# Routing with a running sum of the experts' rounded counts, and other edits around the two routing stages

## The chip, the cores and the metric

The kernel runs on one core of a Trainium2 chip. The metric is the device time of one execution in microseconds (us). A core has TensorE (PE, matmuls; its weight loads are shown as PEld), VectorE (DVE), ScalarE (ACT), GpSimd (POOL) and SyncE (SP), each with its own instruction stream, which meet only at semaphores. The suffix q (DVEq, SPq) marks the sequencer of an engine: register work, branches, waits and DMA issues.

## The reference

Attention for 2 batches x 8 heads with 1152 keys; queries are pooled by two first, so that 576 rows per batch leave it. The result x, 1152 tokens x 512, passes two mixtures of experts:

```python
q_pool = q.reshape(B, H, S // 2, 2, D).mean(axis=3)
attn = softmax(scale * q_pool @ k.T); x = (attn @ v) as [tokens, heads * D]

# first mixture: top-1 of 8 experts, at most cap = 288 tokens for each
logits = x @ w_gate; e = argmax(logits); gate = softmax(logits)[e]
out[i] = gate[i] * (relu(x[i] @ w1[e]) @ w2[e])      # a token past the capacity gives 0

# second mixture: only tokens with x @ w_skip > 0, no capacity
out[i] = x[i] + gate[i] * (relu(x[i] @ w1[e]) @ w2[e])   # other tokens: out[i] = x[i]
```

## The kernel before

Everything is float32, or float32 split in two rounded parts. There are three kinds of stage.

**Attention.** Nine query tiles of 128 rows, head by head. The last head of the loop (`head(H - 1, 1, last=True)`, L852 for PE, L1316 for DVE) ends with the product of probabilities and V in PSUM, which DVE copies to `OT` in one instruction (`copy_output`, L1200); PE turns it back to token rows and takes the gate logits of this head along (`turn_back`, L780); DVE scales both (`output_logits` L1225, `output_x` L1232). `add_logits` (L1244, two reductions) sums the logits over heads, and stands after the last `copy_output`. SP writes each head's columns of x to DRAM with four DMAs (`store_x`, L441: the full tiles and the half tile of either batch), and waits for both of DVE's `output_x` of the head before the first of them.

**Routing, for m = 0 and m = 1** (L857 on PE, L1362 on DVE). Tokens are sorted by expert into tiles of 128 slots. Each expert's share is rounded up to grains of 64 slots, and a tile may hold two experts, so each tile is multiplied by a left and a right expert. DVE makes a one-hot of the expert of each token (`r_hot`). PE counts with it, by triangular and full matrices of ones, the place of every token in its expert and the total of each expert (`pos_ready`). DVE compares the totals with multiples of 64 (`r_cmp`, L1413), sums (`r_nt`), sums again over the experts before (`r_sq`, `r_base`), adds the place, and cuts the slot number in a tile number (`r_which`, `r_tile`) and a row (`r_inside`, `r_place`). POOL multiplies `r_tile` with the token numbers (`r_ids`, L655), PE finds with `r_place` the token of each slot (`rows_found`, L890), DVE writes the row numbers (`rows_in`, L1443), and POOL gathers the first 128 rows of x by an indirect DMA (L606). Beside it DVE and PE find the gates (`r_gcut`, `gates_cut`, L898), and DVE makes the tables of experts per tile (`tab_n`, `tab_done`, `tab_grain`, up to L1464), after which it copies the first right-hand weights (`fill_right`, L323). While PE waits it multiplies `ident` with itself (`keep_busy(n)`, L838, two records for each of the n in the profile).

**Experts** (L986 PE, L1143 ACT, L1481 DVE). For each tile: hidden product, relu, transposes, second product. x comes by POOL's gather, the weights by SP's DMAs of 512 KB in rings of four (first layer) and three (second layer). The row of SP's requests is written by hand: after attention it waits for the last x stores (L463), requests the second-layer weights of expert 0 (L464), waits for the first gathered x tile (L465), and requests more. DVE copies y out for all tiles but the last of m = 0, and takes the logits of the second router from it with nine products (L1355). The last tile of m = 0 goes another way: ACT copies y (L1163), PE turns it (`turn_y`, L975), ACT copies it again (L1165), PE multiplies with the router's weights (`next_logits`, L982), ACT copies the logits (L1167). In the meantime DVE leaves its loop over tiles (L1496, up to 12 passes, of which those past the last tile are skipped by a branch), loads `tab_n` in a register and waits for these logits (L1386). DVE then finds the active tokens, and the routing of m = 1 runs.

Of the kernel before, what the change touches and what calls it, by code (L numbers as in the profile page):

```python
# [37 lines left out]
def build(nc, q, k, v, gate1, w1_1, w2_1, skip_w, gate2, w1_2, w2_2, next_w, out, x_dram, cap):  # L38
# [15 lines left out]
    NCMP = B * SQ // GRAIN  # L54
# [11 lines left out]
    with ExitStack() as ctx:  # L66
# [20 lines left out]
        grain_steps = sb("grain_steps", [P, NCMP])  # L87
        iota_grain = sb("iota_grain", [P, NTAB])
        iota_slot = sb("iota_slot", [P, NSLOT])
        upto = sb("upto", [P, E, E])  # L90
        earlier = sb("earlier", [P, E, E])
# [58 lines left out]
        r_cmp = sb_in(moe, "r_cmp", [P, E, NCMP])  # L150
        r_nt = sb_in(moe, "r_nt", [P, E])
        r_sq = sb_in(moe, "r_sq", [P, E, E])
        r_endc = sb_in(moe, "r_endc", [P, E])
        r_over = sb_in(moe, "r_over", [P, NT, E])
        r_gcut = sb_in(moe, "r_gcut", [P, 2, NSLOT], F32R)
        r_base = sb_in(moe, "r_base", [P, E])
        r_slot = sb_in(moe, "r_slot", [P, NSLOT])
# [3 lines left out]
        r_drop = sb_in(moe, "r_drop", [P, NSLOT])  # L161
# [43 lines left out]
        tile_ready = sem("tile_ready")  # L205
# [21 lines left out]
        CONST_STEPS = 27  # L227
# [131 lines left out]
        def _(sp):  # L359
# [98 lines left out]
            store_x(H - 1)  # L458
# [45 lines left out]
        def _(pool):  # L504
# [60 lines left out]
            for dst, pattern, base in ((expert_rank, [[-1, E]], E), (grain_steps, [[GRAIN, NCMP]], 0),  # L565
                                       (iota_grain, [[1, NTAB]], 0), (iota_slot, [[1, NSLOT]], 0),
                                       (iota_p, [[1, P]], 0)):
                link(nc.gpsimd.iota(dst[:], pattern, base=base, channel_multiplier=0,
                                    allow_small_or_imprecise_dtypes=True))
            link(nc.gpsimd.memset(grain_steps[:, 0:1], -1.0))  # L570
            link(nc.gpsimd.memset(upto[:], 1.0))
            link(nc.gpsimd.affine_select(out=upto[:], in_=upto[:], pattern=[[1, E], [-1, E]], compare_op=ALU.is_ge,
                                         fill=0.0, base=0, channel_multiplier=0))
            link(nc.gpsimd.memset(earlier[:], float(GRAIN)))
            link(nc.gpsimd.affine_select(out=earlier[:], in_=earlier[:], pattern=[[1, E], [-1, E]],
                                         compare_op=ALU.is_gt, fill=0.0, base=0, channel_multiplier=0))
# [11 lines left out]
            for m in range(2):  # L588
# [34 lines left out]
                def store_y(t, count, last=False):  # L623
# [5 lines left out]
                    pool.wait_ge(y_copied, t + 1)  # L629
# [55 lines left out]
        def _(pe):  # L685
# [82 lines left out]
            def turn_back(b, h):  # L768
# [7 lines left out]
                pe.wait_ge(ot_copied, h * 2 + (b + 1))  # L776
# [76 lines left out]
            turn_back(1, H - 1)  # L853

            for m in range(2):
# [15 lines left out]
                pe.matmul(place_of(0, n), before[:], hot, start=True, stop=False, skip_group_check=True)  # L871
                if m == 0:
# [11 lines left out]
                keep_busy((18, 19)[m], HID_BANK + 1)  # L884
# [16 lines left out]
                keep_busy((16, 12)[m], HID_BANK + 1)  # L901
# [70 lines left out]
                def turn_y(t):  # L972
                    pe.wait_ge(y_copied, t + 1)
                    for c in range(DC):
                        mm = pe.transpose(bank(YT_BANK)[:, c * P:(c + 1) * P], ylast[:, c * P:(c + 1) * P], ident[:])  # L975
                    mm.then_inc(y_turned, 1)

                def next_logits():

                    pe.wait_ge(yt_ready, 1)  # L980
                    for c in range(DC):
# [26 lines left out]
                if m == 0:  # L1008
                    keep_busy(2, HID_BANK + 1)
                    turn_y(rest + 1)  # L1010
                    keep_busy(2, HID_BANK + 1)
                    next_logits()
# [3 lines left out]
        def _(act):  # L1016
# [92 lines left out]
            for m in range(2):  # L1109
# [62 lines left out]
        def _(dve):  # L1172
# [21 lines left out]
            def copy_output(b, h):  # L1194
# [5 lines left out]
                nc.vector.tensor_copy(OT[:, b, :], bank(PV_BANK)).then_inc(ot_copied, 1)  # L1200
# [55 lines left out]
            def head(h, par, last=False):  # L1256
# [35 lines left out]
                copy_output(1, h)  # L1292
# [24 lines left out]
            add_logits(0, H)  # L1317
            add_logits(1, H - 1)
# [43 lines left out]
            for m in range(2):  # L1362
# [31 lines left out]
                hot = nc.vector.tensor_tensor(of(r_hot), of(r_rank), per_expert(r_best), ALU.is_equal)  # L1394
                if m == 1:
                    link(hot)
                    hot = nc.vector.tensor_tensor(of(r_hot), of(r_hot), per_expert(active), ALU.mult)
                hot.then_inc(hot_ready, 1)

                if m == 1:  # L1400
                    link(nc.vector.tensor_scalar(r_drop[:], active[:], -float(OUT_OF_RANGE), float(OUT_OF_RANGE),
                                                 ALU.mult, ALU.add))
# [8 lines left out]
                grains = min(-(-cap // GRAIN), NCMP) if m == 0 else NCMP  # L1411
                cmp = r_cmp[:, :, 0:grains]
# [5 lines left out]
                pos = psum[:, 0, 0:n * E].rearrange("p (t e) -> p t e", e=E)  # L1418
                if m == 0:
                    link(nc.vector.tensor_scalar(r_over[:], pos, float(cap), float(OUT_OF_RANGE), ALU.is_ge, ALU.mult))  # L1420
                tt(of(r_pos), pos, per_tile(r_base, E), ALU.add)
                if m == 0:
                    tt(of(r_pos), of(r_pos), r_over[:], ALU.add)
                tt(of(r_pos), of(r_pos), of(r_hot), ALU.mult)
                if m == 0:
                    with nc.allow_low_precision(reason="whole numbers far below 2 ** 24"):
                        reduce(of(r_whole), of(r_pos), ALU.add)
                else:
                    reduce(of(r_slot), of(r_pos), ALU.add)
                    tt(of(r_whole), of(r_slot), r_drop[:], ALU.add)  # L1430
# [112 lines left out]
```

## Time and profile before

| what | us |
|---|---|
| median of 3 runs | 618.69 |
| lowest, highest | 618.34, 618.9 |
| the profiled execution | 618.62 |
| its span, first to last instruction | 616.9 |
| PE busy | 594.9 (96%) |
| DVE busy | 315.1 (51%) |
| ACT busy | 266.9 (43%) |
| mean share of full TensorE clock granted | 0.995 |

Times in the views count from the first instruction. Attention ends on PE near 273 us, the first routing lasts to about 291 us, the experts of m = 0 to 446.6 us, the second routing to 466.5 us, and the experts of m = 1 to the end. A row that says busy tells how long the engine had an instruction in work, not that the end of the kernel depends on it.

### The profile page before, as it was taken

What the parts mean: (1) busy time and instruction counts of PE and PEld (TensorE: products, weight loads), DVE (VectorE), ACT (ScalarE), POOL (GpSimd) and SP (SyncE); (2) the same over time, 40 slices, a digit from 0 to 9 for tenths busy, and PEclk for the clock granted to TensorE, in tenths of its full rate; (3) what the DMA queues carried; (4) which work ended last, traced back from release to release, by engine and by line L of the source; (5) the groups of instructions that cost most, each with busy time, mean ns of one, the idle gap of its engine ahead of it and who ended that gap; (6) DMA issues with size and microseconds to landing.
All of it is one profiled execution on the core that took longest, in us unless ns stands there. A gap on an engine that the chain in (4) does not pass through costs nothing.

```text
span 616.9 us, 12447 instructions
## 1 busy us (share of the span) xinstructions
PE 594.9 (96%) x3719; PEld 352.3 (57%) x3720; DVE 315.1 (51%) x666; ACT 266.9 (43%) x439; POOL 191.5 (31%) x168
## 2 busy tenths in 40 slices
PE   8899999999999999998999999999999999999993
PEld 7677787877777777777333333333395333333331
DVE  5457565657575756656355652965574220322220
ACT  4655565655565656520244444444102444444410
POOL 4785635344453800001012221122211122222222
PEclk9999999999999999999999999999999999999997
DMA  8979818171721062006999397780846798841111
GB/s 201 291 184 258 186 39 173 39 166 45 153 50 26 11 232 87 22 9 208 399 391 409 124 352 275 284 307 29 305 174 229 274 312 322 321 150 43 45 52 61
DMA packets 42637, 111.61 MB, mean 181 GB/s; under 512 B 16020, under 2 KB 16020, under 8 KB 41536
## 3 DMA queue, kind: packets, MB, share of 16 engines
q1 hardware_dynamic: 38528, 99.03, 50.5%
q0 software_dynamic: 4080, 12.22, 5.7%
q8 instruction: 15, 0.25, 0.2%
q14 instruction: 14, 0.11, 0.1%
HBM read 102.68 MB, written 12.06 MB: 186 GB/s over the span
## 4 chain that ended last, share of the span: by engine, by line
PE 90%; DMA 2%; DVE 2%; issue 2%; ACT 2%; POOLq 0%; POOL 0%; SPq 0%; DVEq 0%; ACTq 0%
PE psum L929 41%; PE psum L704 14%; PE psum L718 11%; PE psum L752 9%; PE psum L916 4%; PE psum L838 3%; PE psum L780 3%; PE psum L764 1%; PE psum L748 1%; DMA xraw<-moe_in,rows_in 1%; DVE probs L1181 1%; ACT probs L1019 1%; PE psum L931 1%; DMA qraw<-in_q_dram 1%; DMA res<-moe_in,idx_r 1%
## 5 line engine op out<-in xcount | busy, mean ns | idle before, releaser
L929 PE MATMUL psum<-w1ring,XT 128*64 x304 | 134.5, 595 | 0.8 <-ACT XT L1126 0.4
L929 PE MATMUL psum<-w2ring,HT 128*64 x304 | 133.7, 592 | 1.7 <-DVE wright L323 1.7
L931 PE MATMUL psum<-wright,XT 128*64 128x512 f32 x304 | 134.5, 595 | 0.0
L931 PE MATMUL psum<-wright,HT 128*64 128x512 f32 x304 | 133.7, 592 | 0.0
L1181 DVE TENSOR_SCALAR_CACHE_REDUCE probs<-psum 128x1152 f32<-128x1152 f32 x72 | 97.5, 1357 | 62.6 <-PE psum L704 62.6
L1019 ACT ACTIVATE probs<-probs,nmax 128x1152 f32<-128x1152 f32 x72 | 90.7, 1260 | 45.6 <-DVE probs L1181 45.6
L704 PE MATMUL psum<-KT,QT 128*128 128x384 f32 x480 | 102.0, 350 | 3.0 <-DVE probs L1181 1.7
L929 PEld LDWEIGHTS psum<-w2ring,HT 128*64 128x64 f32 x304 | 41.5, 137 | 87.3 <-issue 87.3
L704 PEld LDWEIGHTS psum<-KT,QT 128*128 128x128 f32 x480 | 80.2, 188 | 15.0 <-issue 7.9
L929 PEld LDWEIGHTS psum<-w1ring,XT 128*64 128x64 f32 x304 | 40.1, 137 | 79.8 <-issue 79.8
L718 PE MATMUL psum<-ident,probs 128*128 128x128 f32 x648 | 82.0, 275 | 1.1 <-ACT probs L1019 0.6
L718 PEld LDWEIGHTS psum<-ident,probs 128*128 128x128 f32 x648 | 72.7, 140 | 9.2 <-issue 3.7
L1133 ACT ACTIVATE hid<-psum,slot_gate 128x1024 f32<-128x1024 f32 x19 | 21.2, 1114 | 125.2 <-PE psum L931 125.2
L1026 ACT COPY PT<-psum 128x512 f32<-128x512 f32 x88 | 48.4, 588 | 60.3 <-PE psum L718 60.3
L752 PE MATMUL psum<-PT,V 128*64 128x512 f32 x256 | 62.2, 605 | 0.0
L323 ACT COPY wright<-w1ring 128x1024 f32 x60 | 58.1, 1040 | 0.0
L323 DVE COPY wright<-w2ring 128x1024 f32 x76 | 49.1, 700 | 14.3 <-DMA w2ring<-in_moe_w_dram 14.2
L1348 DVE TENSOR_TENSOR orow<-psum,res 128x512 f32<-128x512 f32 x9 | 6.2, 691 | 97.0 <-PE psum L931 88.1
L1355 DVE CUSTOM_DVE_ANT_0 psum<-ysb,wnext 128x512 f32<-128x512 f32 x81 | 52.9, 723 | 0.0
L595 POOL COPY idx_x<-rows_in 128x1 int32 x15 | 8.8, 585 | 142.0 <-PE psum L916 142.0
L335 POOL CAST KT<-kraw 128x2304 fp32r<-128x2304 f32 x7 | 14.7, 2106 | 87.3 <-PE psum L704 82.8
L931 PEld LDWEIGHTS psum<-wright,HT 128*64 128x64 f32 x304 | 41.5, 137 | 0.0
(169 smaller groups left out, 645.7 us busy)
## 6 DMA issues: line engine op xcount, KB each, us to landing
w1ring<-in_moe_w_dram SPq DMA_DIRECT2D x64, 512.0 KB, 6.9
w2ring<-in_moe_w_dram SPq DMA_DIRECT2D x64, 512.0 KB, 7.1
qraw<-in_q_dram SPq DMA_DIRECT2D x30, 288.0 KB, 10.0
kraw<-in_k_dram SPq DMA_DIRECT2D x14, 576.0 KB, 9.2
V<-in_v_dram SPq DMA_DIRECT2D x8, 576.0 KB, 4.0
moe_in<-zero SPq DMA_DIRECT2D x9, 256.0 KB, 3.1
wnext<-in_next_w_dram SPq DMA_DIRECT2D x1, 2304.0 KB, 17.1
out_dram<-moe_in SPq DMA_DIRECT2D x1, 2304.0 KB, 9.4
```

Source lines behind the costliest of these rows:

```text
L323: copy(wright[k][:, part * PIECE:(part + 1) * PIECE], piece_of(k, slot, part).rearrange("p o f -> p (o f)")).then_inc(filled, 1)
L704: mm = pe.matmul(dst, QT[par][:, piece, q0:q0 + P], KT[par][:, b * S + c * KB:b * S + (c + 1) * KB], start=(i == 0), stop=(i == 2 * len(pa ...
L718: mm = pe.transpose(bank(T_BANK + place % 3)[:, i * P:(i + 1) * P], src, ident[:])
L752: mm = pe.matmul(psum[rows, PV_BANK, :], V[par][:, b * KT_N + j, :], PT[:, j, :], start=(j < 2), stop=False, skip_group_check=True)
L916: return pe.matmul(place[:, chunk * P:(chunk + 1) * P], src, ident[:], is_transpose=True, start=first, stop=False, skip_group_check=True)
L929: pe.matmul(psum[0:GRAIN, b, :], lhs[:, c * P:c * P + GRAIN], left, start=first, stop=last, skip_group_check=True)
L931: return pe.matmul(psum[GRAIN:P, b, :], lhs[:, c * P + GRAIN:(c + 1) * P], wright[k][:, cols], start=first, stop=last, skip_group_check=True)
L1019: nc.scalar.activation(probs[:, t, :], probs[:, t, :], ACT.Exp, bias=nmax[:, t:t + 1], scale=-1.0, accum_out=den[:, t:t + 1]).then_inc(pro ...
L1026: nc.scalar.copy(dst, bank(T_BANK + place % 3, cols)).then_inc(turned_by_act, 1)
L1133: nc.scalar.activation(hid[:].rearrange("p (c f) -> p c f", c=2), psum[:, HID_BANK:HID_BANK + 2, :], ACT.Relu, scale=g).then_inc(relu_read ...
L1181: nc.vector.tensor_scalar(probs[:, t, :].rearrange("p (c k) -> p c k", c=3), scores_in(h, t), -SCALE, None, ALU.mult, ALU.min, accum_out=n ...
L1355: nc.vector.tensor_tensor_reduce(out=bank(JUNK_BANK + e % 2), in0=ysb[:], in1=wnext[:, e, :], scale=1.0, scalar=0.0, op0=ALU.mult, op1=ALU ...
```

## The change

The grain count is rounded by float arithmetic: `half_grain` adds 31.5 to each expert's total on PE, and a running sum (`tensor_tensor_scan`) that starts at ROUND + P, where neighbouring floats are 64 apart, gives the rounded ends of all experts in one instruction. `grain_steps`, `upto`, `earlier` and the arrays made from them are gone. Capacity is cut by a mask on the one-hot; slots are counted from P, so that a token that is left out gets 0 and meets no tile. Five counts of `keep_busy` shrink. The last head's `OT` is copied in two halves, three of the four last x stores are issued when their rows are written, the last y tile is copied in halves, and DVE instead of ACT copies the turned y and its logits. SP's requests after the x stores are as before: the second-layer weights of expert 0 come ahead of the wait for the first x.

```diff
-            store_x(H - 1)
+            last_rows = token_rows(x_dram[0])
+            for i, written in ((0, 2 * H - 1), (1, 2 * H - 1), (3, 2 * H - 1), (2, 2 * H)):
+                sp.wait_ge(x_written, written)
+                parts, tiles, rows = last_rows[i]
+                sp.dma_start(rows[:, :, (H - 1) * D:H * D], xpair[parts, tiles, :]).then_inc(x_stored, 16)
...
-                    pool.wait_ge(y_copied, t + 1)
+                    if last:
+                        pool.wait_ge(ylast_copied, 2)
+                    else:
+                        pool.wait_ge(y_copied, t + 1)
...
+                if last:
+                    pe.wait_ge(ot_part, 1)
+                else:
+                    pe.wait_ge(ot_copied, h * 2 + (b + 1))
...
+                    if last and n == 2:
+                        pe.wait_ge(ot_copied, h * 2 + (b + 1))
...
+                pe.matmul(place_of(n, n + 1), whole[:], half_grain[:].unsqueeze(1), start=False, stop=False, skip_group_check=True)
...
-                keep_busy((18, 19)[m], HID_BANK + 1)
+                keep_busy((14, 14)[m], HID_BANK + 1)
...
-                keep_busy((16, 12)[m], HID_BANK + 1)
+                keep_busy((8, 8)[m], HID_BANK + 1)
...
+                def turn_y():
+
+                    for i in range(2):
+                        pe.wait_ge(ylast_copied, i + 1)
+                        for c in range(2 * i, 2 * i + 2):
+                            mm = pe.transpose(bank(YT_BANK + i)[:, c * P:(c + 1) * P], ylast[:, c * P:(c + 1) * P], ident[:])
+                        mm.then_inc(y_turned, 1)
+
+                def next_logits():
+
                     for c in range(DC):
+                        if c % 2 == 0:
+                            pe.wait_ge(yt_ready, c // 2 + 1)
                         mm = pe.matmul(bank(LG_BANK, E + 1), yT[:, c * P:(c + 1) * P], wcat[:, c, :],
...
-                    nc.scalar.copy(ylast[:], bank(Y_BANK)).then_inc(y_copied_[0], 1)
-                    act.wait_ge(y_turned, 1)
-                    nc.scalar.copy(yT[:], bank(YT_BANK)).then_inc(yt_ready, 1)
-                    act.wait_ge(lg_done, 1)
-                    nc.scalar.copy(logits2[:, bass.ds(rest + 1, 1), :].rearrange("p o c -> p (o c)"), bank(LG_BANK, E + 1)
-                                   ).then_inc(lg_copied, 1)
+                    for i in range(2):
+                        half = slice(i * 2 * P, (i + 1) * 2 * P)
+                        nc.scalar.copy(ylast[:, half], bank(Y_BANK)[:, half]).then_inc(ylast_copied, 1)
...
+                if last:
+                    add_logits(0, H)
+                    add_logits(1, H - 1)
+                copy_output(1, h, last)
...
-                    link(nc.vector.tensor_scalar(active[:], logits2[:, :, E], 0.0, None, ALU.is_gt))
+                    nc.vector.tensor_scalar(active[:], logits2[:, :, E], 0.0, 2.0 * E, ALU.is_gt, ALU.mult).then_inc(active_ready, 1)
...
-                if m == 1:
-                    link(hot)
-                    hot = nc.vector.tensor_tensor(of(r_hot), of(r_hot), per_expert(active), ALU.mult)
+                if m == 0:
+                    hot = nc.vector.tensor_tensor(of(r_hot), of(r_rank), per_expert(r_best), ALU.is_equal)
+                else:
+                    dve.wait_ge(active_ready, 1)
+                    tt(of(r_best), of(r_best), active[:], ALU.add)
+                    hot = nc.vector.scalar_tensor_tensor(of(r_hot), of(r_rank), 2.0 * E, per_expert(r_best), ALU.add, ALU.is_equal)
...
-                tt(cmp, bc(tot.unsqueeze(2), [P, E, grains]), bc(grain_steps[:, 0:grains].unsqueeze(1), [P, E, grains]), ALU.is_gt)
-                reduce(r_nt[:], cmp, ALU.add)
-                tt(r_sq[:], bc(r_nt[:].unsqueeze(1), [P, E, E]), earlier[:], ALU.mult)
-                reduce(r_base[:], r_sq[:], ALU.add)
+                half = (GRAIN - 1) / 2.0
+                link(nc.vector.tensor_scalar(r_held[:], tot, float(cap if m == 0 else B * SQ) + half, 1.0 + half, ALU.min, ALU.max))
+                link(nc.vector.tensor_tensor_scan(ends[:, 1:E + 1], r_held[:], r_held[:], ROUND + P, ALU.add, ALU.max))
...
-                    link(nc.vector.tensor_scalar(r_over[:], pos, float(cap), float(OUT_OF_RANGE), ALU.is_ge, ALU.mult))
-                tt(of(r_pos), pos, per_tile(r_base, E), ALU.add)
+                    nc.vector.scalar_tensor_tensor(of(kept), pos, float(cap), of(r_hot), ALU.is_lt, ALU.mult).then_inc(kept_ready, 1)
+                link(nc.vector.scalar_tensor_tensor(of(r_pos), per_tile(ends[:, 0:E], E), ROUND, pos, ALU.subtract, ALU.add))
...
-                    reduce(of(r_slot), of(r_pos), ALU.add)
-                    tt(of(r_whole), of(r_slot), r_drop[:], ALU.add)
-                link(nc.vector.tensor_scalar(of(r_inside), of(r_whole), P - 1, None, ALU.bitwise_and))
+                nc.vector.tensor_scalar(of(r_inside), of(r_whole), P - 1, None, ALU.bitwise_and).then_inc(inside_ready, 1)
...
+                if m == 0:
+                    sum_gates()
                 dve.wait_ge(rows_found, m + 1)
                 found = psum[:, 7, 0:NSLOT]
                 nc.vector.tensor_scalar(rows_in[m][:, 0:NSLOT], found, -1.0, 0.0, ALU.add, ALU.max).then_inc(rows_in_ready, 1)
-                if m == 0:
-                    sum_gates()
...
-                tt(r_sq[:], bc(r_nt[:].unsqueeze(1), [P, E, E]), upto[:], ALU.mult)
-                reduce(r_endc[:], r_sq[:], ALU.add)
...
-                if m == 1:
+                if m == 0:
+                    for i in range(2):
+                        half = slice(i * 2 * P, (i + 1) * 2 * P)
+                        dve.wait_ge(y_turned, i + 1)
+                        nc.vector.tensor_copy(yT[:, half], bank(YT_BANK + i)[:, half]).then_inc(yt_ready, 1)
+                    at = bass.ds(rest + 1, 1)
+                    dve.wait_ge(lg_done, 1)
+                    nc.vector.tensor_copy(logits2[:, at, :].rearrange("p o c -> p (o c)"), bank(LG_BANK, E + 1)
+                                          ).then_inc(lg_copied, 1)
+                else:
                     copy_y(m, rest + 1)
```

## Rows read from the trace of the kernel before

**Rows 1.** The page's chain that ended last: share of the span by engine.

```profile
PE 90%; DMA 2%; DVE 2%; issue 2%; ACT 2%; POOLq 0%; POOL 0%; SPq 0%; DVEq 0%; ACTq 0%
```

**Rows 2.** Chain of waits through the first routing: start us, us, what.

```profile
271.61 0.70 DVE OT L1200
...
273.53 2.50 PE psum L838 x22
...
276.41 4.12 PE psum L838 x36
...
283.05 6.28 DMA xraw<-moe_in,rows_in
```

**Rows 3.** Timeline of DVE, first routing: start us, us, engine, line, what, xcount.

```profile
269.49 0.48 DVE L1232 TENSOR_TENSOR xpair<-psum,rden 128x320 f32<-128x320 f32 x1
...
274.42 0.23 DVE L1390 TENSOR_TENSOR r_diff<-logits,r_max 128x72 f32<-128x72 f32 x1
274.57 0.23 DVE L1335 TENSOR_TENSOR r_eq<-logits,r_max 128x72 f32<-128x72 f32 x1
...
276.45 0.20 DVE L1335 TENSOR_TENSOR r_cmp<-psum,grain_steps 128x40 f32<-128x40 f32 x1 [0.51 <-PE psum L867]
...
279.38 1.70 DVE L1437 TENSOR_TENSOR r_place<-iota_p,r_inside 128x384 fp32r<-128x384 f32 x3
...
281.94 0.22 DVE L1338 TENSOR_REDUCE r_sum<-r_exp 128x9 f32<-128x72 f32 x1
...
282.65 0.17 DVE L1446 CAST r_gcut<-gate 128x9 fp32r<-128x9 f32 x1
...
287.20 2.50 DVE L323 COPY wright<-w1ring 128x1024 f32 x4 [1.37 <-issue]
```

**Rows 4.** Timeline of SP, first routing: the last x stores, the weight request.

```profile
275.96 3.27 SPq L441 DMA_DIRECT2D moe_in<-xpair  x4
280.61 0.36 SPq L397 DMA_DIRECT2D w2ring<-in_moe_w_dram  x1
```

**Rows 5.** DMA issues, 275.9 to 276.1, then 277.9 to 278.6: us to landing last.

```profile
moe_in<-xpair SPq DMA_DIRECT2D x1, 128.0 KB, 2.0
...
moe_in<-xpair SPq DMA_DIRECT2D x1, 128.0 KB, 3.3
```

**Rows 6.** Chain of waits through the second routing.

```profile
448.59 1.06 PE psum L982 x8
...
452.89 4.35 PE psum L838 x38
...
462.46 2.77 PE psum L838 x24
```

**Rows 7.** Timeline of DVE, second routing.

```profile
449.98 0.17 DVE L1387 TENSOR_SCALAR active<-logits 128x14 f32<-128x14 f32 x1 [3.21 <-ACT logits L1167]
...
453.09 0.31 DVE L1335 TENSOR_TENSOR r_cmp<-psum,grain_steps 128x144 f32<-128x144 f32 x1
...
456.11 2.61 DVE L1437 TENSOR_TENSOR r_place<-iota_p,r_inside 128x384 fp32r<-128x384 f32 x5
```

**Rows 8.** DVE's sequencer, 446 to 450: count, ns, first and last start us.

```profile
L1496 DVEq ALU_OP  x5: 40/40/40, 446.6 to 448.9; - x5
L1386 DVEq TENSOR_LOAD <-tab_n x1: 317/317/317, 449.0 to 449.0; - x1
L1386 DVEq ALU_OP  x1: 40/40/40, 449.7 to 449.7; - x1
```

**Rows 9.** POOL's first gather of m = 1, and its us to landing.

```profile
460.59 1.08 POOL L606 DMA_INDIRECT xraw<-moe_in,rows_in  x1 [3.56 <-DVE rows_in L1443]
xraw<-moe_in,rows_in POOLq DMA_INDIRECT x1, 3.5
```

**Rows 10.** Windows after the last matmul: stretch, length, busy, PEclk, DMA share, GB/s.

```profile
607.00:608.00 1.00, 0.07 (x2) 0.00 (x0) 0.00 (x0) 0.00 (x0) 0.30 (x2) 1.00 0.35 49
...
610.50:611.00 0.50, 0.00 (x0) 0.00 (x0) 0.00 (x0) 0.00 (x0) 0.00 (x0) 0.68 0.00 0
```

More of the change, by code:

```diff
@@ L53, in build @@
     NSLOT = -(-NGRAIN // (2 * PER_TILE)) * 2
-    NCMP = B * SQ // GRAIN
+    ROUND = float(GRAIN * 3 << 22)
     KB = S // 3
@@ L86, in build @@
         expert_rank = sb("expert_rank", [P, E])
-        grain_steps = sb("grain_steps", [P, NCMP])
+        half_grain = sb("half_grain", [P, E], BF16)
+        ends = sb("ends", [P, E + 1])
         iota_grain = sb("iota_grain", [P, NTAB])
         iota_slot = sb("iota_slot", [P, NSLOT])
-        upto = sb("upto", [P, E, E])
-        earlier = sb("earlier", [P, E, E])
         wcat = sb("wcat", [P, DC, E + 1])
@@ L149, in build @@
         r_pos = sb_in(moe, "r_pos", [P, NSLOT, E])
[L150 to L154, printed above, removed]
+        r_held = sb_in(moe, "r_held", [P, E])
+        r_kept = sb_in(moe, "r_kept", [P, NT, E])
         r_gcut = sb_in(moe, "r_gcut", [P, 2, NSLOT], F32R)
-        r_base = sb_in(moe, "r_base", [P, E])
-        r_slot = sb_in(moe, "r_slot", [P, NSLOT])
         r_whole = sb_in(moe, "r_whole", [P, NSLOT], I32)
@@ L225, in build @@
         res_loaded = sem("res_loaded")
-        CONST_STEPS = 27
+        CONST_STEPS = 23
         START = 1
@@ L564, in _ @@
             link(nc.gpsimd.tensor_copy(into_upper[:], scratch[:]))
-            for dst, pattern, base in ((expert_rank, [[-1, E]], E), (grain_steps, [[GRAIN, NCMP]], 0),
-                                       (iota_grain, [[1, NTAB]], 0), (iota_slot, [[1, NSLOT]], 0),
+            for dst, pattern, base in ((expert_rank, [[-1, E]], E), (iota_grain, [[GRAIN, NTAB]], P),
+                                       (iota_slot, [[1, NSLOT]], 1),
                                        (iota_p, [[1, P]], 0)):
@@ L569, in _ @@
                                     allow_small_or_imprecise_dtypes=True))
[L570 to L576, printed above, removed]
+            link(nc.gpsimd.memset(half_grain[:], (GRAIN - 1) / (2.0 * P)))
+            link(nc.gpsimd.memset(ends[:, 0:1], ROUND + P))
             for b in range(B):
@@ L766, in attend_mid, with turn_back @@
                 mm.then_inc(mid_done, 1)
-            def turn_back(b, h):
+            def turn_back(b, h, last=False):
                 if b == 0:
@@ L852, in _ @@
             head(H - 1, 1, last=True)
-            turn_back(1, H - 1)
+            turn_back(1, H - 1, last=True)
             for m in range(2):
@@ L1192, in copy_tiles, with copy_output @@
                     copy_turned(h, turn_no(b, j))
-            def copy_output(b, h):
+            def copy_output(b, h, last=False):
                 u = h * 2 + b
@@ L1291, in head @@
                     maximum(h + 1, 3)
-                copy_output(1, h)
+                if last:
+                    add_logits(0, H)
+                    add_logits(1, H - 1)
+                copy_output(1, h, last)
             nc.vector.memset(qraw[0][:, :, SQ:SQ + P], 0.0).then_inc(pads_ready, 1)
@@ L1425, in _ @@
-                if m == 0:
-                    with nc.allow_low_precision(reason="whole numbers far below 2 ** 24"):
-                        reduce(of(r_whole), of(r_pos), ALU.add)
-                else:
-                    reduce(of(r_slot), of(r_pos), ALU.add)
-                    tt(of(r_whole), of(r_slot), r_drop[:], ALU.add)
-                link(nc.vector.tensor_scalar(of(r_inside), of(r_whole), P - 1, None, ALU.bitwise_and))
+                    dve.wait_ge(kept_ready, 1)
+                tt(of(r_pos), of(r_pos), of(kept), ALU.mult)
@@ L1432, in _ @@
+                with nc.allow_low_precision(reason="whole numbers far below 2 ** 24"):
+                    reduce(of(r_whole), of(r_pos), ALU.add)
+                nc.vector.tensor_scalar(of(r_inside), of(r_whole), P - 1, None, ALU.bitwise_and).then_inc(inside_ready, 1)
                 link(nc.vector.tensor_scalar(of(r_which), of(r_whole), 7, None, ALU.logical_shift_right))
@@ L1452, in _ @@
                 last.then_inc(gates_cut, 1)
-                tt(r_sq[:], bc(r_nt[:].unsqueeze(1), [P, E, E]), upto[:], ALU.mult)
-                reduce(r_endc[:], r_sq[:], ALU.add)
-                link(nc.vector.tensor_scalar(r_ends[:], r_endc[:], float(PER_TILE - 1), None, ALU.add))
-                link(nc.vector.tensor_scalar(r_tiles[:], r_ends[:], SHIFT, None, ALU.logical_shift_right))
+                link(nc.vector.tensor_scalar(r_ends[:], ends[:, 1:E + 1], ROUND + P, float(P - 1), ALU.subtract, ALU.add))
+                link(nc.vector.tensor_scalar(r_tiles[:], r_ends[:], 7, None, ALU.logical_shift_right))
                 link(nc.vector.tensor_scalar(tab_n[m][:], r_tiles[0:1, E - 1:E], -2.0, None, ALU.add))
-                tt(r_til[:], bc(iota_grain[:].unsqueeze(2), [P, NTAB, E - 1]),
-                   bc(r_endc[:, 0:E - 1].unsqueeze(1), [P, NTAB, E - 1]), ALU.is_ge)
+                link(nc.vector.scalar_tensor_tensor(r_til[:], bc(ends[:, 1:E].unsqueeze(1), [P, NTAB, E - 1]), ROUND,
+                                                    bc(iota_grain[:].unsqueeze(2), [P, NTAB, E - 1]),
+                                                    ALU.subtract, ALU.is_le))
                 reduce(r_tab[:], r_til[:], ALU.add)
```

34 lines of the change are left out of this document (11 added, 23 removed).

## The prediction

> **What bounds the kernel now.** I read the chain of waits first. PE holds 90% of it [rows 1], so an edit counts only where it lets PE go on earlier. The experts' stages are unbroken products and the diff leaves them alone; what it touches lies in the two routings. Next I read the chain through each of them. In the first it goes from DVE's last copy of the attention output at 271.61 over PE's filler (`keep_busy`, L838) to the first gather of x, 6.28 us from issue to landing, at 283.05 + 6.28 = 289.33 [rows 2]. In the second it is filler and small products throughout: 38 filler records to 452.89 + 4.35 = 457.24 and 24 more to 462.46 + 2.77 = 465.23 [rows 6]. There the gather landed at 460.59 + 3.5 = 464.1, before PE wanted it [rows 9]. So the first routing ends with a transfer, the second with a count of filler matmuls. One filler costs two records, 2 x 4.12 / 36 = 0.229 us [rows 2].
>
> Each routing is walked through below in times of the old trace.
>
> **First routing up to the gather.** (a) DVE copied `OT` from 271.61 in 0.70. Halves of 256 columns are not in the trace; 320 columns from PSUM took 0.48 [rows 3], and a line through 0.70 and 0.48 gives 0.41. PE can start after the first half, 0.70 - 0.41 = 0.29 earlier; I take 0.28. The bounds are 0, if a half cost as much as the whole, and 0.35. `add_logits`, moved ahead of the copy, falls in DVE's wait from 269.49 + 0.48 = 269.97 to 271.61. The turn and the 11 fillers that follow move with it, and so do the x rows of the last half head.
>
> (b) The one matmul of 8 columns for `half_grain` I take at 0.03, within 0 to 0.2. PE's totals come 0.25 earlier, so DVE's first operation on them stands at 276.20 in place of 276.45.
>
> (c) From there to the first `r_place` DVE took 279.38 - 276.45 = 2.93 [rows 3] for twelve small operations, nearly all waiting for the one before. An unlinked pair stands 0.15 apart (274.42, 274.57) and a linked one costs its duration and some 0.04. Now there are nine: the clamp 0.21, the scan, the mask 0.15 unlinked, place plus base 0.27, times mask 0.27, sum 0.26, `r_inside` 0.10 unlinked, `r_which` 0.21, `r_tile` 0.21. No row shows a scan. It has 8 elements; the nearest row, 40 elements of `r_cmp`, took 0.20, and 72 elements 0.23, so 0.25 with its link, bounds 0.2 and 0.6. Sum 1.93. `r_place` starts at 278.13.
>
> (d) PE had used `r_place` 1.15 after its start (276.41 + 4.12 = 280.53 against 279.38). With 14 fillers for 18 it comes free at 276.16 + 3.21 = 279.37, 1.24 after the new start, so the shorter filler uncovers nothing. `rows_found` is 1.16 earlier. `sum_gates`, 282.65 - 281.94 = 0.71 long [rows 3], goes into DVE's wait for it. POOL issues the gather at 283.05 - 1.17 = 281.88.
>
> **What the gather then waits for.** (e) The x stores: all four were issued from 275.96, over 3.27 us, and SP requested weights at 280.61, when the last had landed [rows 4]. The first full tile, issued with nothing ahead of it, landed in 2.0, a later one in 3.3 [rows 5]. Now three go out from 269.97 and have 5.7 us for it; only the last full one follows `output_x` at 275.96 - 0.28 = 275.68. With 2.0 it lands at 277.7, and the weight request moves to 277.75: 2.86 earlier (by 3.3: 1.6 earlier).
>
> (f) The weights' 2 MB and the gather's 0.26 MB fill the queues together until the gather lands, 289.33 - 280.61 = 8.72 after the first request. The gather alone needed 3.5 [rows 9]; the other 2.8 of its 6.28 is this traffic. If it still lands when all of it has drained, x is there at 277.75 + 8.72 = 286.5. If the queues shared fully, or the weights were gone, it lands at 281.88 + 3.5 = 285.4. The weights have been under way 4.1 us when the gather is issued, against 2.4 before, so a little less of them is in front: I take 286.3, 3.0 earlier.
>
> (g) PE's filler after the gates falls from 16 to 8 and ends near 284.7; PE then stands idle some 1.6 us until x comes. DVE's first weight copy started at 287.20 [rows 3]. It moves by 1.17 + 0.71 at least, to 285.3, and its first quarter (0.63) is ready at 285.9, before XT can be used near 287.9. The first hidden product is 3.0 earlier. The experts' weights are requested when x lands or when a ring slot is free; these requests move along.
>
> **Second routing.** (h) The turned y. Before, ACT copied it and PE's eight product records began at 448.59 and took 1.06 to 449.65 [rows 6]. Now DVE copies it, and DVE isn't there in time: its sequencer goes through the skipped passes of the loop over tiles until 448.9 + 0.1 = 449.0 [rows 8], a time set by the nine products with the last but one y and not by anything that the change shortens. It hid behind ACT's path; now it is the path. The copy of the first half goes 449.08 to 449.50, the second to 449.83; PE's products run from 449.54 in two halves of 0.53 to 450.60, 0.95 late. That ACT hands y over in halves gains nothing ahead of such a wait.
>
> (i) The register load. `tab_n` is loaded for the wait on the logits, from 449.0 to 449.74 [rows 8]; before, this too lay ahead of the logits, which came at 449.95. Now the load stands in program order behind DVE's own wait for PE and its copy. Copy at 450.70, load done at 451.44, `active` at 451.52 instead of 449.98 [rows 7]: 1.54 late. If the sequencer went on to the load without waiting, (i) would shrink to about 0.75.
>
> (j) From `active` to PE's totals took 452.89 - 449.98 = 2.91. `active` unlinked saves 0.1, one addition over 14 elements for a product over 112 saves 0.1, the extra matmul costs 0.03: 2.74, totals at 454.26, 1.37 late. `r_drop` is gone, so DVE, which came 0.20 after PE (453.09), is there with it, at 454.30. Its chain was 456.11 - 453.09 = 3.02 [rows 7] and is 0.21 + 0.25 + 0.31 + 0.31 + 0.30 + 0.10 + 0.21 + 0.28 = 1.97 by the same pricing: `r_place` at 456.27, 0.16 late. Fourteen fillers take PE from 454.26 to 457.47, 0.23 late; that covers `r_place` by 1.20 where it had 1.13.
>
> (k) The gather is issued at 460.59 + 0.23 = 460.82 and lands by 464.3. The gates' products end 0.23 late, at 462.69; 8 fillers for 12 take 1.85, to 464.54. That is 0.7 before 465.23. The gather is 0.2 ahead of it, so it isn't late. DVE's tables lose two operations and hold nothing up.
>
> **Sum.** 3.0 + 0.7 = 3.7 us. Against the profiled execution's 618.62 (span 616.9 and 1.7 around it; 0.07 below the median of the runs) this is 614.9 us. A difference of 0.2%, 1.2 us, is about what a measurement of this kernel can tell from none.
>
> **Rivals.** *The gather shares instead of draining.* x lands at 285.4, the first part gains 3.9, time 614.0. For it: most of the weights are gone by then. Against it: before, 0.26 MB took 2.8 us longer than alone and landed last. The Trainium skill ("DMA: Bandwidth & Descriptors", Queues, rings and completion order) has each engine alternate packet by packet between its queues, which is this rival's rule; the old trace doesn't bear it out as equal shares.
>
> *The stores land late.* If the last x store takes 3.3, the weights start 1.6 earlier only and x lands with them, at 287.7: 1.6 + 0.7 = 2.3, time 616.3. For it: the 3.3 of [rows 5]. Against it: that one was issued behind others.
>
> *DVE is in time.* If (h) and (i) cost nothing, the filler counts and the gather bound the second routing: everything to the gather's issue is 1.3 earlier, and x lands at 462.8, 2.3 before 465.2. Time 613.3. Against it: the loop's end at 449.0 is read, not assumed.
>
> *The clock falls (the slower side).* PE idles 1.6 us ahead of x, or up to 3.0 if the filler ends early and x comes at 287.7, where 16 fillers once bridged all but 0.9. After the last matmul the granted clock stayed at full speed from 607.1 to about 610.5 [rows 10], so 3.4 us of idling did not lower it there; this idle is shorter. If it does fall to 1.2 GHz, the first hidden product, 7.1 us, runs at half pace: 3.5 us if it recovers half way, 7 if not; with 5, 619.9. It decides from an added loss of 3.7. The Trainium skill ("TensorE: Matmul & The Clock Gate", HAM oscillation) names just such waits for a transfer between bursts as what brings the clock down; by it alone one would leave the fillers in. Rows 10 speak against it for this length.
>
> **How the numbers follow.** Forecast, 613.9 to 616.0 with its own errors: 0.55. Sharing gather 0.1, DVE in time 0.07, late stores 0.16, clock 0.07. The remaining 0.05 is for a loss I don't see, such as a scan at its upper bound together with a later ylast store, ending near no change. The forecast's unknowns, scan 0.2 to 0.6 twice, halves 0 to 0.35, reach to 616; with the late stores 617.0 is the upper end, with the other two 613.3 the lower. The first three and most of the late stores are faster by more than 1.2 us: 0.81. Within 0.2%: 0.11. Slower: 0.08.
>
> **What would show it.** In the profile after: SP's weight request near 277.8 (e); `r_place` 1.9 after the first operation on the totals (c); the first gather landing near 286.3, with PE idle ahead of it and a clock of 1.00 (f, g); DVE's copy of the turned y near 449.1 less 3.0, idle PE ahead of the products, and the load of `tab_n` behind the copy of the logits (h, i), each in the new trace's times; PE without a wait for x in the second routing (k). The distance from the last y product of m = 0 (446.6) to the second routing's end (465.2), 18.6 us, should be 17.9. The prediction is wrong if x lands with the weights unchanged, if the distance grows, or if a clock below 1.00 stands behind 284.

## The result

The changed kernel takes 619.70 us in the median of 13 runs (618.77 to 622.34), the kernel before 618.67 (617.99 to 619.81): ratio 1.0021, 95% interval 1.0011 to 1.0031. It is slower by 1.0 us where 3.8 less were forecast. The profiled execution took 618.77 us with a span of 617.0 and is the fastest of the 13. The mean granted clock is 0.988 to 0.993 in these runs, against 0.995 in the profiled execution before.

The chain of waits through the first routing, which answers to [rows 2]:

```profile
271.54 0.43 DVE OT L1204
...
273.19 2.50 PE psum L840 x22
...
276.10 3.23 PE psum L840 x28
...
281.85 6.46 DMA xraw<-moe_in,rows_in
...
290.02 1.05 PE psum L932
...
298.45 1.12 ACT hid L1139
```

The gather is issued 1.20 us earlier and still takes 6.46 us. The first matmul record of the hidden product is 1.05 long, where it was 0.64 before. PE's first instruction on x, and then the windows of this stretch (length, busy time of PE, PEld, DVE, ACT, POOL, then granted clock, DMA share, GB/s):

```profile
288.36 0.65 PE L919 MATMUL psum<-ident,xraw 128*128 128x128 f32 x4 [3.62 <-DMA xraw<-moe_in,rows_in]
...
284.00:285.00 1.00, 0.74 (x7) 0.55 (x5) 0.34 (x1) 0.00 (x0) 0.00 (x0) 1.00 1.01 401
...
287.00:288.00 1.00, 0.00 (x0) 0.00 (x0) 0.86 (x6) 0.00 (x0) 0.00 (x0) 1.00 0.47 189
288.00:289.00 1.00, 0.64 (x6) 0.65 (x7) 0.24 (x2) 0.00 (x0) 0.00 (x0) 1.00 0.00 0
289.00:290.00 1.00, 1.00 (x9) 0.78 (x7) 0.00 (x0) 0.65 (x2) 0.08 (x1) 0.59 0.63 119
...
291.00:292.00 1.00, 1.00 (x6) 0.34 (x4) 0.00 (x0) 0.00 (x0) 0.00 (x0) 0.50 0.88 307
292.00:293.00 1.00, 1.00 (x4) 0.16 (x2) 0.00 (x0) 0.00 (x0) 0.00 (x0) 0.70 1.00 410
```

PE ran out of fillers at 284.74 and stood idle for 3.62 us until x landed at 288.31. The clock then stood at 1.2 GHz from near 289.2 to 292.6, and the first hidden product lasted from 289.95 to 298.36, 8.4 us where it took 7.1 before. It begins 0.98 earlier and its end is 0.33 later than before, not 3.0 earlier.

DVE's chain, beside [rows 3], is as fast as hoped:

```profile
276.13 0.17 DVE L1418 TENSOR_SCALAR r_held<-psum 128x8 f32<-128x8 f32 x1 [0.54 <-PE psum L869]
276.33 0.18 DVE L1419 TENSOR_TENSOR_SCAN ends<-r_held 128x8 f32<-128x8 f32 x1
...
277.96 1.70 DVE L1439 TENSOR_TENSOR r_place<-iota_p,r_inside 128x384 fp32r<-128x384 f32 x3
```

SP and the last x store, beside [rows 4, 5]: the timeline, then the DMA issue of 275.6 to 276.4, then the packets of the hardware queue and of the instruction queue from 277.0 to 277.5, the instruction queue alone from 277.45 to 277.5, then the packets from 277.5 to 279.6.

```profile
269.92 6.08 SPq L457 DMA_DIRECT2D moe_in<-xpair  x4
279.79 10.38 SPq L392 DMA_DIRECT2D w2ring<-in_moe_w_dram  x8
...
moe_in<-xpair SPq DMA_DIRECT2D x1, 128.0 KB, 4.0
...
q1 hardware_dynamic: 132, 0.03, 27.1%
q8 instruction: 1, 0.02, 11.6%
...
q8 instruction: 1, 0.02, 116.0%
...
q1 hardware_dynamic: 33, 0.01, 3.1%
```

The last store landed 4.0 us after its issue, with no other store ahead of it. Of its 528 packets 495 had gone by 277.5; the other 33 came after 278. 528 packets over 16 DMA engines are 33 for each, so one engine's whole share was late. One packet of the instruction queue (a fetch of instructions, by the queue's name) began at 277.49. A share of 116.0% of 16 engines in 0.05 us is 0.93 us for it, so that it ended at 278.42; the first of the 33 late packets began at 278.40.

The second routing, DVE beside [rows 7, 9], then PE's wait for DVE's copy:

```profile
449.21 0.76 DVE L1504 COPY yT<-psum 128x256 f32<-128x256 f32 x2 [2.26 <-issue]
450.93 0.17 DVE L1507 COPY logits<-psum 128x9 f32 x1 [0.97 <-PE psum L988]
451.69 0.17 DVE L1395 TENSOR_SCALAR active<-logits 128x14 f32<-128x14 f32 x1 [0.59 <-DVE logits L1507]
...
456.56 2.62 DVE L1439 TENSOR_TENSOR r_place<-iota_p,r_inside 128x384 fp32r<-128x384 f32 x5
...
449.69 1.06 PE L988 MATMUL psum<-wcat,yT 128*128 128x9 f32 x8 [1.34 <-DVE yT L1504]
```

The last y product of m = 0 ends 0.14 later than before, so DVE's copy and `active` stand where they were forecast. PE waited 1.34 us for the copy; the clock stayed at 1.00 there. x landed 3.8 us after POOL's issue at 461.06, and PE turned it at 464.90: 0.17 earlier than before, from a start 0.14 later. The hidden product of m = 1 starts at 466.42, 0.13 earlier than before. By the end of the execution 0.3 us is lost again, and where was not followed up.

### The profile page after: what moved, and what is told of

The parts are those of the page before. It is cut to its first block, busy times and chain, and to the rows that moved or that the text cites. A ratio compares the mean times of both kernels' runs of the same rounds, so it can differ in the third digit from the quotient of the medians.

```text
span 617.0 us, 12355 instructions
## 1 busy us (share of the span) xinstructions
PE 591.3 (96%) x3679; PEld 348.0 (56%) x3680; DVE 312.1 (51%) x659; ACT 266.1 (43%) x438; POOL 190.6 (31%) x164
## 4 chain that ended last, share of the span: by engine, by line
PE 88%; DVE 4%; issue 3%; DMA 2%; ACT 2%; DVEq 0%; POOLq 0%; POOL 0%; SPq 0%; ACTq 0%
PE psum L932 40%; PE psum L701 14%; PE psum L715 11%; PE psum L749 9%; PE psum L919 4%; PE psum L782 3%; PE psum L840 2%; PE psum L761 1%; PE psum L745 1%; DMA xraw<-moe_in,rows_in 1%; DVE probs L1184 1%; ACT probs L1025 1%; PE psum L934 1%; DMA qraw<-in_q_dram 1%; DMA res<-moe_in,idx_r 1%
```

## The experiments

All times are medians; each ratio is against the kernel before, run on the same chip. Differences from the changed kernel are taken between medians of different chips; the kernel before had 618.56 to 618.70 on them.

**Fillers against the clock.** The changed kernel with 16:

```diff
-                keep_busy((8, 8)[m], HID_BANK + 1)
+                keep_busy((16, 8)[m], HID_BANK + 1)
```

> The changed kernel with 16 fillers instead of 8 behind the gates of m = 0 (8 stay for m = 1). Theory A, the clock: PE idled 3.6 us ahead of the first x, the clock fell to 1.2 GHz and the first hidden product took 8.4 us for 7.1. With 16 fillers the idle is 1.8 us, the clock stays at 1.00, x lands where it did, near 288.3: about 1.4 us less than the changed kernel, near 618.2 when before stands at 618.7. Rival B, the fillers don't matter and the whole change is a wash because the gather comes with the weights: same time as the changed kernel, 619.7, and the spread of its runs stays as wide.

618.33 us, ratio 0.9994 (0.9985 to 1.0003), 1.4 less than the changed kernel. The size is as expected, the reason isn't: PE idled only 1.93 us and the clock fell all the same, from 288.9. The two profiled executions, which both lost it, took the same time (618.75 and 618.77), so where the 1.4 of the medians comes from is not shown.

```profile
289.00:290.00 1.00, 1.00 (x6) 0.96 (x5) 0.00 (x0) 0.65 (x2) 0.12 (x1) 0.50 0.91 147
...
292.00:293.00 1.00, 1.00 (x8) 0.36 (x6) 0.00 (x0) 0.00 (x0) 0.00 (x0) 0.87 1.03 418
```

**The same cut in the kernel before**, 16 to 8 for m = 0 and nothing else:

```diff
-                keep_busy((16, 12)[m], HID_BANK + 1)
+                keep_busy((8, 12)[m], HID_BANK + 1)
```

> The kernel before with one number changed: 8 fillers instead of 16 behind the gates of m = 0. x still lands near 289.3, so PE idles some 2.7 us ahead of it. Theory A1, the clock falls after any idle of this kind: first hidden product 1.0 to 1.4 us longer, time 619.9. Theory A2, an idle of 2.7 us is still short enough and only the 3.6 of the changed kernel lost the clock: same time as before, 618.7, clock 1.00 through the stage. Which one holds tells whether the fillers alone, without the rest of the change, cost the time.

620.13 us, 1.0022 (1.0011 to 1.0033). PE idled 3.13 us ahead of x, and the clock was low from 290.4 to 293.9. Theory A1 holds: this number alone makes the kernel slower by as much as the whole change does. Of the 1.8 us by which the profiled execution is longer, 0.5 is no clock: x landed at 289.80 for 289.33. Of its 12 runs the two with a mean clock of 0.996 and 0.997 took 617.96 and 618.50; those at 0.989 took 621.2 to 621.8.

```profile
289.85 0.66 PE L916 MATMUL psum<-ident,xraw 128*128 128x128 f32 x4 [3.13 <-DMA xraw<-moe_in,rows_in]
```

**Enough fillers**, 24 in the changed kernel:

```diff
-                keep_busy((8, 8)[m], HID_BANK + 1)
+                keep_busy((24, 8)[m], HID_BANK + 1)
```

> The changed kernel with 24 fillers instead of 8 behind the gates of m = 0, enough to reach from 282.7 to the first x at 288.3 (8 left 3.6 us idle and 16 left 1.9, and both lost the clock). Theory A: the loss of the change lies in this idle alone; clock 1.00 to the tail, first hidden product 7.1 us for 8.4, and besides no run with a long low stretch: 617.6 to 618.1, with a spread under 1 us where the changed kernel has 3.6. Rival B: the clock is lost in the second routing's idle instead (PE waits 1.3 us for DVE's copy of the turned y), or something else takes the gain: 619 and more, wide spread.

618.01 us, 0.9994 (0.9986 to 1.0003), runs from 616.92 to 619.24. In the first routing theory A came true (clock 1.00 through, hidden product from 289.75). But rival B is right of the whole: now the clock fell in the second routing, behind PE's 1.34 us of waiting for DVE's copy of the turned y, and 11 fillers took 4.1 us for 2.7. From the turning of y (L980) to the hidden product of m = 1 it is 20.0 us, in the changed kernel's trace 19.2.

```profile
448.00:450.00 2.00, 1.74 (x11) 1.74 (x12) 0.71 (x3) 0.00 (x0) 0.00 (x0) 0.75 0.30 115
450.00:452.00 2.00, 2.00 (x11) 2.00 (x11) 1.36 (x6) 0.30 (x1) 0.00 (x0) 0.50 1.24 393
452.00:454.00 2.00, 2.00 (x29) 1.99 (x28) 1.05 (x5) 0.00 (x0) 0.00 (x0) 0.90 0.99 369
```

**ACT copies the turned y** and its logits in the changed kernel, halves kept:

```diff
-                        nc.vector.tensor_copy(yT[:, half], bank(YT_BANK + i)[:, half]).then_inc(yt_ready, 1)
...
+                        nc.scalar.copy(yT[:, half], bank(YT_BANK + i)[:, half]).then_inc(yt_ready, 1)
```

> The changed kernel with the two halves of the turned y and the logits of the last tile of m = 0 copied by ACT, as before, instead of by DVE. Theory A: DVE's late arrival and its register load cost some 1.5 us between the last y product of m = 0 and the second routing's active tokens; without them active stands near 450.1, place finding comes 1.5 us earlier, and the time falls by 1.3 to 1.5 us to near 618.3. The clock in m = 0 is still lost. Rival B, the fillers (14 and 8) and not DVE bound the second routing, so that the gain is under 0.5 us: 619.3.

617.03 us, 0.9976 (0.9966 to 0.9985): 2.7 less than the changed kernel, more than the 1.5 expected. In the trace the products start at 448.03 without a wait, and the hidden product of m = 1 at 464.37 for 466.42, 2.0 earlier. The clock was lost in the first routing and kept in the second, as in the changed kernel's trace, so these 2.0 are path. `active` began at 449.77, though ACT had the logits at 449.29; the register load stood between, and the next run takes this load out of the changed kernel.

**Without the second load of `tab_n`**:

```diff
-                    dve.wait_ge(lg_copied, dve.value_load(tab_n[0][:], min_val=0, max_val=NSLOT - 2) + 2)
+                    dve.wait_ge(lg_copied, rest + 2)
```

> The changed kernel with one register load taken away: DVE's wait for the last logits of m = 0 uses the register that already holds the tile count, instead of loading tab_n again. Theory A: the load stands on the path behind DVE's own copy of the logits (0.76 us from that copy to active in the changed kernel), so active comes 0.5 to 0.6 us earlier and the time falls by as much, to near 619.1. Rival B, DVE's late arrival (the loop's skipped passes) is all that counts and the load is hidden by the copy's completion: no difference, 619.7.

618.09 us, 1.0001 (0.9989 to 1.0013). `active` follows the copy of the logits by 0.20 instead of 0.76, which is theory A, and the two profiled executions differ by 0.73. The median fell by 1.6; the runs lie in two groups (617.2 to 618.1, and 619.3 to 621.1), so the rest may be the clock's chance; it was not followed up.

```profile
451.06 0.17 DVE L1395 TENSOR_SCALAR active<-logits 128x14 f32<-128x14 f32 x1
```

**Both repairs with 24 fillers**, weights still ahead of x:

> The same, with the turned y and its logits copied by ACT and without the second load of tab_n: the changed kernel with the weights still requested ahead of the first x, and its two faults taken out. Theory A: the first routing as in the version with 24 fillers, the second as in the version with all three repairs: hidden product 17.9 us after the last y product of m = 0 (442.95 to 460.85 there) for 19.8, so 1.9 us less than with 24 fillers alone: near 615.8. It lies 2.4 above the version with x first (613.4), which is what the transfer order is worth with the clock held.

614.98 us, 0.9947 (0.9934 to 0.996), runs within 0.6 us, clock 1.00 up to the last product. The gain over 24 fillers alone is 3.0, of which 1.9 was expected. In the traces the way from the turning of y to the hidden product of m = 1 is 2.9 shorter (17.05 for 19.96): 2.2 against the changed kernel's 19.22, and the other 0.7 is the clock of the second routing.

**The order of the requests.** First x, then weights, in the changed kernel:

```diff
-            load_matrix(SECOND, 0, 0)
             sp.wait_ge(x_loaded_[0], 16)
+            load_matrix(SECOND, 0, 0)
```

> The changed kernel with SP waiting for the first x before it requests the second-layer weights of expert 0, so that nothing is on the queues beside the gather. Theory A: x lands 3.5 to 3.8 us after POOL's issue, near 285.5, PE's idle shrinks to under 1 us with only 8 fillers, the clock stays at 1.00: 2.8 us earlier plus 1.3 of clock, near 615.6. Rival B, the gather is slow of itself in this stage: it lands 6.3 us after its issue as before and the time stays near 619.7. Rival C, the weights come too late for the first y product: a wait of PE on the second right-hand weights of 1 to 3 us takes part of it back, 617 to 618.

615.94 us, 0.9949 (0.9936 to 0.9962). x landed 3.8 us after its issue, PE idled 0.91 and the clock stayed at 1.00 there; PE waited for no weights. It fell in the second routing instead, as with 24 fillers, after the same wait of 1.34 us. Of its five runs the two at a mean clock of 0.994 took 614.6 and 614.9, the others 615.9 to 616.5.

The same edit in the kernel before:

> The kernel before with one edit: SP waits for the first x before it requests the second-layer weights of expert 0. Theory A, the gather's wait behind the weights is 2.5 to 2.8 us there as well: x lands near 286.8, but PE's 16 fillers run until 288.5, so that only 0.9 of it can be taken: 617.8, clock 1.00. Rival B, the gain is the same 3.8 us that this edit brought to the changed kernel (619.7 to 615.9), 614.9: then the fillers are no bound. It tells how much of that 3.8 was transfer and how much was clock.

617.23 us, 0.9974 (0.9962 to 0.9986): 1.3 less, where theory A gave 0.9 (of its 3.8 in the changed kernel, the rest is fillers that no longer bound and clock). Its 11 runs lie within 0.4 us.

**All three repairs** (x first, ACT's copies, no second load):

> The changed kernel with the three repairs together: the first x ahead of the weights, ACT copies the turned y and its logits, and no second load of tab_n. Theory A: they add up, 3.8 for the first (615.9 alone), 2.7 for the second (617.0 alone), and 0.5 for the third, since in the version with ACT's copies DVE's active was still held by the load (449.77, logits there at 449.29): 619.7 - 3.8 - 2.7 - 0.5 = 612.7. Rival B: part of both gains is the same clock regained, and they overlap: 614.

613.39 us, 0.9916 (0.9903 to 0.993), runs within 0.3 us: faster than both kernels by more than 5 us. The parts overlapped by 0.7, between the two theories. PE idled 0.88 us ahead of the first x and the clock stayed. With 12 fillers for 14 behind the totals of both routings besides:

> The version with the three repairs, with 12 fillers instead of 14 behind the totals in both routings. PE reaches the token products 1.1 to 1.2 us after the first r_place begins, and POOL's r_ids is ready 0.8 after it. Theory A: both gathers are issued 0.4 us earlier and nothing else bounds, 0.6 to 0.8 in all: 612.7. Rival B: r_place is made at 0.52 us for three tiles where PE uses them at 0.49, so PE catches up with it in the second routing, or x comes no earlier: under 0.3, 613.2.

613.16 us, 0.9913 (0.9901 to 0.9926), no difference that can be told from 613.39; rival B. PE waited 1.36 us for the first x without losing the clock, and in the second routing 0.4 us for POOL's `r_ids` and 0.6 for x.

**The last x store.** The early stores alone, in the kernel before, with the same edit of the stores as in the change:

> The kernel before with the x stores of the last head issued early, as in the change, and nothing else. Theory A, the last store lands not 2 but 3.7 to 4 us after its issue at 275.96, because a fetch of instructions (one packet of the instruction queue near 277) holds one of the 16 DMA engines and this engine's share of the store comes 2 us after the others: weights requested near 279.9, 0.7 earlier, the gather at 283.05 as before and landing 0.3 to 0.7 earlier, time 618.2 to 618.7. Rival B, the store lands after 2.0 us, as the same transfer did with nothing ahead of it: weights requested near 278.1, x 2 us earlier but PE's fillers until 288.5: 617.8.

617.74 us, 0.9985 (0.9976 to 0.9994). The store landed in 3.3 us, with 33 late packets and an instruction packet at 277.31; weights were requested at 279.65 and the hidden product began at 290.07 for 290.93. That is theory A's mechanism; the gain of 0.8 is more than its 0.5 and as much as rival B's.

Then PE's and DVE's programs were lengthened in the changed kernel, to move the fetch of instructions:

```diff
+            for _ in range(60):
+                pe.sem_inc(settled, 1)
             pe.wait_ge(consts_ready, 1)
...
+            for _ in range(60):
+                dve.sem_inc(settled, 1)
             nc.vector.memset(qraw[0][:, :, SQ:SQ + P], 0.0).then_inc(pads_ready, 1)
```

> The changed kernel with 60 semaphore increments more at the start of PE's and of DVE's program, so that both programs' later instructions lie a quarter of an instruction page further on; some 2 us later at the start, and the time itself says nothing. Theory A: the 2 us by which 33 packets of the last x store come after the rest are due to the packet of the instruction queue at 277, and this fetch is PE's or DVE's: it now comes some us earlier, away from the store, and the store lands 2.0 us after its issue, with no late packets. Rival B: the late packets have nothing to do with the fetch, or the fetch is another engine's: fetch and store keep their distance and the store lands after 3.4 to 4.0.

One execution, 623.35 us, 7.5 us later throughout this stretch. The instruction packet now passed between 281 and 282.2, before the store was issued near 283.2. Of this kernel: that packet, the store's packets and landing, SP's weight request, PE's first use of x, and PE's wait for DVE's copy in the second routing.

```profile
q8 instruction: 1, 0.02, 6.7%
...
q1 hardware_dynamic: 528, 0.13, 26.2%
...
moe_in<-xpair SPq DMA_DIRECT2D x1, 128.0 KB, 2.0
...
285.22 10.53 SPq L392 DMA_DIRECT2D w2ring<-in_moe_w_dram  x8
...
293.94 0.66 PE L921 MATMUL psum<-ident,xraw 128*128 128x128 f32 x4 [1.71 <-DMA xraw<-moe_in,rows_in]
...
454.97 1.06 PE L990 MATMUL psum<-wcat,yT 128*128 128x9 f32 x8 [1.90 <-DVE yT L1508]
```

No packet was late, the store landed in 2.0 us, and the gather took 4.56 us instead of 6.46. From the end of `output_x` to the first hidden product it is 12.4 us (283.09 to 295.52), in the changed kernel 14.4 (275.60 to 289.95). PE idled 1.71 and the clock stayed at 1.00; it also stayed at 1.00 behind the wait of 1.90 in the second routing. Theory A holds. Whether PE's or DVE's fetch it was stays open, both were moved.

The other thirteen traces (both kernels and eleven experiments) bear it out. In each an instruction packet began between 276.59 and 277.49 and took 0.93 to 1.63 us, and the first late store packet came within 0.02 us of its end. In the ten traces with the early stores 33 packets were late and the last store landed after 3.2 to 4.0 us. In the kernel before and its versions with 8 fillers and with x first 38 were late. What kept the late engine from its packets before the instruction packet began is not shown.

## Why the prediction was wrong

**(a) to (d), right.** The halves took 0.42 each (0.41 forecast) and PE began 0.34 earlier; DVE's first operation stood at 276.13 (276.20), its chain took 1.83 (1.93), the scan 0.18 (0.25 with its link), the gather was issued at 281.85 (281.88).

**(e), the step that failed.** The last store took 4.0 us, not 2.0, and the weights were requested at 279.79, not 277.75: 0.8 earlier for 2.86. I had taken the 3.3 of [rows 5] for queueing behind other stores. It was queueing, but behind one late engine's share of them, which comes whether other stores stand ahead or not. Of the kernel before: all four issues, then the packets from 278.2 to 279.15, and from 279.15 to 280.2:

```profile
L441 SPq DMA_DIRECT2D moe_in<-xpair x4: 372/524/1718, 276.0 to 278.7; - x4
...
q1 hardware_dynamic: 38, 0.01, 7.4%
...
q1 hardware_dynamic: 608, 0.15, 62.5%
```

The store of 3.3 us was already issued from 276.9 on, which took 1.72 us, and its packets began when the last of the 38 late ones ahead had gone. In the changed kernel the late share was the last store's own. Where the fetch was moved away, 2.0 came true, and (f) with it: 4.56 us for the gather against the 4.4 that I took.

**(f) and (g), wrong by what (e) left.** With the weights 2.06 us ahead of the gather (4.1 forecast, 2.4 before) the gather drained with them: 288.31, where the draining case gives 279.79 + 8.72 = 288.5. The gain was 1.0 of 3.0. The sharing rival is refuted for this spacing.

**The clock rival came true**, at a chance of 0.07. That its 619.9 stands so near the measured 619.7 is luck: it priced the slow clock at 5 us with x 3.0 earlier, and in the trace x was 1.0 earlier and the slow clock cost 1.3. The late stores and the clock, two rivals told apart in the prediction, came together. The fillers were cut by as much as a gain of 3.0 would allow, so the missing 2.0 became idle time. I judged it by the idle after the last matmul, 3.4 us at full clock [rows 10], as if the length alone decided. It doesn't: 3.1 to 3.6 and 1.93 us ahead of x lost the clock, 1.71, 1.36 and 0.91 kept it. Nor does the place alone: in the second routing 1.34 us behind the same instructions lost it in two traces (24 fillers, and x first) and kept it in three (the changed kernel, 16 fillers, no second load), and the padded kernel kept it there through 1.90. What decides stays open, and the tail was no measure of it. The Trainium skill ("TensorE: Matmul & The Clock Gate", HAM oscillation) warns of waits for a transfer between bursts; these traces agree (3.62 us ahead of x lost it), and they lost the clock after shorter idles too, 1.93 and 1.34 us.

**(h) and (i), right.** DVE's late arrival and the load behind it cost what was said: copy at 449.21 (449.08 and 0.14 of shift), `active` at 451.69 (451.52 and 0.14). What I missed is what PE's idle does there: it puts the clock at risk a second time, and a loss there costs 0.7 to 0.9 us more by the two traces that show one (20.0 and 20.2 us from the turning of y to the hidden product, for 19.2). ACT's copies are worth 2.0 by the path alone, since with halves `active` comes 1.9 earlier; that the rest of the median's 2.7 is this clock is likely and not shown.

**(j) and (k), mis-sized.** `r_place` came 0.15 later than forecast beside the shift, the addition of `active` having waited 0.19; x took 3.8 us for 3.5 and landed with the end of the fillers, and the hidden product then waited 0.20 for DVE's weight copy. The gain there was 0.3, not 0.7.

The profiled execution lost 0.15 us on the old one, the median 1.0. The other runs have mean clocks of 0.988 to 0.993, all but one below the profiled 0.992. A second loss, in the second routing, would fit in size (0.7 to 0.9 us). But none of these runs has a trace, and no trace shows both losses: the three that waited 1.34 us with the clock lost in the first routing kept it in the second. Where these 0.9 us go stays open.

## What to carry to other kernels

A filler count belongs to the transfer that it bridges: cut it only after the transfer has been seen to land earlier, and don't put a change that should bring a gain and a cut that spends the gain in one edit. An engine that is idle in the profile may still be late, if its sequencer has a loop to leave or a register to load; read its sequencer's rows before giving it work on the path. Before a store's time to landing is taken over to another place, count its packets: a share of one sixteenth that comes late points to one DMA engine, and other stores ahead needn't be the reason.

## What the runs showed of the hardware

One 16 KB packet of the instruction queue can hold back a DMA engine's share of a store by 1 to 2 us, and with it everything that waits for the store's completion (3.2 to 4.0 us to landing with it, 2.0 without). It moved with 60 instructions of padding in each of two programs. That the granted clock fell after 1.93 us of idle and after 1.34, but not after 1.71 and 1.90 in another trace, was unexpected, and so was where the time went: with 24 fillers, and with x first, the clock kept in the first routing was lost in the second, with no change made there.
